# Moving a 16-column GpSimd copy behind eight other instructions, and ScalarE's wait for it to the end of the previous window, in an attention, FFT and FFN kernel

## What is computed

```python
def _moe_ref(x, w_ch1, w_ch2):
    X = np.fft.fft(x, axis=1)
    X = np.fft.fft(X, axis=2)
    mixed = np.real(X).astype(np.float32)
    u = x + mixed
    ...
    un = (u - mu) / np.sqrt(var + 1e-06)
    ch = np.maximum(un @ w_ch1, 0.0) @ w_ch2
    return (u + ch).astype(np.float32)

def _moe2_ref(x, w_val, conv_w, w_out):
    ...
    for k in range(K):
        gate_pre += conv_w[k][None, None, :] * xp[:, k:k + S, :]
    gate = 1.0 / (1.0 + np.exp(-gate_pre))
    val = x @ w_val
    return (gate * val @ w_out).astype(np.float32)
```

## Time and profile before

| | us |
|---|---|
| median of 3 runs | 617.36 |
| lowest and highest | 616.98, 617.66 |
| the profiled execution | 616.98 |
| its span | 615.2 |
| TensorE busy in the span | 604.8 (98%) |
| VectorE, ScalarE, GpSimd busy | 425.7, 345.6, 342.0 |

### The profile page before, as it was taken

One profiled execution on the slowest core, in us unless ns is written; L12 is line 12 of the kernel. 1 busy time (PEld: TensorE's weight loads), 2 busy tenths in 40 slices (PEclk: granted clock), 3 DMA queues, 4 the chain that ended last, 5 costly groups with the idle time before them and its releaser, 6 DMA issues.

```text
span 615.2 us, 10882 instructions
## 1 busy us (share of the span) xinstructions
PE 604.8 (98%) x3682; PEld 502.5 (82%) x3682; DVE 425.7 (69%) x683; ACT 345.6 (56%) x694; POOL 342.0 (56%) x328
## 2 busy tenths in 40 slices
PE   6899999999999999999999999999999999999998
PEld 3667777777767776999888899999999999988887
DVE  3978888888888885788475566655676666579920
ACT  4877777777777785354444344435444444274242
POOL 4543433333337756146325798883999999234140
PEclk9999999999999999999999999999999999999999
DMA  6942323233233110000321212123222221100102
GB/s 146 235 118 64 91 66 90 69 86 90 67 86 92 49 59 7 0 2 2 103 68 52 69 41 67 62 61 99 69 85 85 85 84 53 35 0 1 69 34 103
DMA packets 28177, 42.21 MB, mean 69 GB/s; under 512 B 3440, under 2 KB 16240, under 8 KB 28144
## 3 DMA queue, kind: packets, MB, share of 16 engines
q1 hardware_dynamic: 26176, 37.38, 20.7%
q0 software_dynamic: 1728, 4.02, 2.7%
q10 hardware_dynamic: 240, 0.39, 0.3%
HBM read 38.63 MB, written 3.15 MB: 68 GB/s over the span
## 4 chain that ended last, share of the span: by engine, by line
PE 95%; DVE 2%; ACT 1%; DMA 1%; POOL 1%; issue 0%; SPq 0%; ACTq 0%; POOLq 0%
PE banks L1876 22%; PE banks L1908 14%; PE banks L1663 12%; PE banks L1680 11%; PE banks L1730 10%; PE banks L1867 6%; PE banks L1990 5%; PE banks L2006 5%; PE banks L1703 2%; PE banks L1813 2%; PE banks L1616 2%; PE banks L1738 1%; PE banks L1853 1%; DMA q_raw<-in_q 1%; PE banks L1622 1%; PE banks L1787 1%
## 5 line engine op out<-in xcount | busy, mean ns | idle before, releaser
L1242 DVE TENSOR_REDUCE row_min<-banks 128x1 f32<-128x768 f32 x96 | 91.8, 956 | 32.0 <-PE banks L1663 31.2
L872 ACT ACTIVATE prob<-banks,row_min 128x768 f32<-128x768 f32 x96 | 87.0, 906 | 29.3 <-DVE row_min L1242 29.2
L1730 PE MATMUL banks<-ident,prob 128*128 128x128 f32 x576 | 79.2, 273 | 1.5 <-ACT probT L374 1.4
L1502 DVE TENSOR_TENSOR partial_sums<-banks,partial_sums 128x384 f32<-128x384 f32 x72 | 40.1, 557 | 50.6 <-PE banks L1908 50.5
L1730 PEld LDWEIGHTS banks<-ident,prob 128*128 128x128 f32 x576 | 68.1, 140 | 6.7 <-issue 1.9
L1680 PE MATMUL banks<-probT,v_in 128*64 128x384 f32 x384 | 69.0, 495 | 0.0
L605 POOL TENSOR_TENSOR k_b<-k_raw,k_a 64x768 fp32r<-64x768 f32 x16 | 29.2, 1827 | 69.9 <-ACT k_a L855 69.8
L1876 PE MATMUL banks<-h_hi,w_hi 128*128 128x512 f32 (+1 forms) x256 | 66.1, 339 | 0.0
L1876 PE MATMUL banks<-h_hi,w_lo 128*128 128x512 f32 (+1 forms) x256 | 65.6, 337 | 0.0
L1876 PE MATMUL banks<-h_lo,w_hi 128*128 128x512 f32 (+1 forms) x256 | 65.4, 337 | 0.0
L374 ACT COPY probT<-banks 128x384 f32<-128x384 f32 x104 | 49.0, 479 | 22.5 <-PE banks L1730 22.2
(11 more groups left out here) (216 smaller groups left out, 1511.3 us busy)
## 6 DMA issues: line engine op xcount, KB each, us to landing
w_stage<-in_moe_w_ch SPq DMA_DIRECT2D x40, 256.0 KB, 2.6
q_raw<-in_q SPq DMA_DIRECT2D x32, 192.0 KB, 3.3
k_raw<-in_k SPq DMA_DIRECT2D x30, 192.0 KB, 3.6
v_in<-in_v SPq DMA_DIRECT2D x16, 192.0 KB, 2.8
w_pair<-in_moe_w_ch SPq DMA_DIRECT2D x6, 512.0 KB, 3.8
w_stage<-in_moe_w_ch SPq DMA_DIRECT2D x6, 512.0 KB, 3.8
out<-y_out SPq DMA_DIRECT2D x11, 256.0 KB, 2.0
seq_tables_sb<-in_dft POOLq DMA_DIRECT2D x6, 386.0 KB, 3.7
```

Of the source, the lines that this page charges most:

```text
L872: act.activation(prob[s % 2][:, :, :], s_tile(s), ACT.Exp, bias=row_min[:, s:s + 1], scale=-1.0, accum_out=row_sum[:, s:s + 1]).then_inc(e ...
L1242: dve.tensor_reduce(row_min[:, s:s + 1], s_tile(s), AX.XY, ALU.min).then_inc(min_ready, 1)
L1502: dve.tensor_tensor(out, product_bank[PRODUCT_BANK[o]], other, ALU.add).then_inc(done, 1)
L1730: op = pe.transpose(bank[:, j * P:(j + 1) * P], prob[tile % 2][:, c, j * P:(j + 1) * P], ident[:, :])
```

## The change

On GpSimd, in window 4 (g == SEAM), `finish_x2(0)` is moved from behind the first `split_w2` to behind the second one. In between lie three `split_w1_pair`, the four sums of `sum_w1_pair` and one `split_w2`. On ScalarE, three waits that stood in window 5 ahead of `first_tap(0, 0)` now stand at the end of window 4, which is ahead of `copy_first(5)`. No instruction that computes is added or removed.

```diff
                 split_w2(PLAIN + 2 * g, 0)
-                if g == SEAM:
-                    finish_x2(0)
                 if more:
                     for o in range(4, 7):
                         split_w1_pair(g + 1, o)
                 if g + 2 < WINDOWS:
                     sum_w1_pair(g + 2)
                 split_w2(PLAIN + 2 * g + 1, 1)
+                if g == SEAM:
+                    finish_x2(0)
                 if g > SEAM:
                     split_wvo(g - SEAM - 1)
...
                 copy_first(g)
                 if more:
                     round_w1_pair(g + 1, 0)
-                if g == SEAM + 1:
-                    act.wait_ge(taps_spread, 2)
-                    act.wait_ge(x2_lead, 2)
-                    act.wait_ge(unsum_lo_done, 8)
                 if g > SEAM:
                     first_tap(0, g - SEAM - 1)
...
                 split_w2(PLAIN + 2 * g + 1, 1, PLAIN // 2 + g + 1)
                 if SEAM < g <= SEAM + KB:
                     round_x2(0, slice(g - SEAM - 1, g - SEAM))
+                if g == SEAM:
+                    act.wait_ge(taps_spread, 2)
+                    act.wait_ge(x2_lead, 2)
+                    act.wait_ge(unsum_lo_done, 8)
```

## The result

The changed kernel takes 625.07 us (624.51 to 625.20) against 617.32 us (616.98 to 617.66) before: a ratio of 1.0124, 95% interval 1.0106 to 1.0141, so 7.75 us more. Both are medians of four runs; the 617.36 above is that of three. The prediction was 621.5 us, with a range of 620.7 to 624.4: the direction was right, the time lies above the range. The profiled execution of the changed kernel took 624.13 us, its span is 622.5 us.

The account below looks back on a forecast made before the run. TensorE, busy 98% of the span, was taken as the bound. Copy end 435.09 plus a 1.16 us chain, less 432.07, gave a 4.18 us stall; on the 617.36 median 621.54, forecast 621.5 us, range 620.7 to 624.4.

Parts of the forecast that it names:

- The place, the chain and the sign: Window 4 to 5: late GpSimd copy delays copy_first(5), VectorE's first addition, then TensorE's product 2; slower, chance 0.95.
- The gap: TensorE ahead of product 2 of window 5: stands still 4.18 us, from 432.07 to 436.25; bounds 3.50 and 5.07.
- The handoff from ScalarE to VectorE: Between copy_first(5) and VectorE's first addition of window 5: 0.04 us, estimated from another handoff.
- No second stall: Product 3 of window 5: its addition ends at 438.16, before 438.36; no second wait, or at most 0.2 us.
- The clock: TensorE behind the idle time in window 5: clock taken as unchanged, no loss added to the forecast; chance 0.62.
- rival 1: TensorE behind the idle time in window 5: clock falls to the lower level, 1.9 us more, 623.5 us; chance 0.28.
- Its price: Lower clock behind the idle time: half of 3.78 us lost, 1.9 us; with the late bound 7.0 us, 624.4 us.
- Rival 2: GpSimd runs the eight instructions ahead of the copy in about 5 us; stall about 2 us, 619.4 us; chance 0.06.
- Rival 3: The late copy still meets its wait in time; no slower, 617.0 to 617.4 us; chance 0.04.
- The date that I gave for it: Product 2 of window 5 is on time if GpSimd's copy ends by 432.07 - 1.16 = 430.91 us.

Follow-up runs that it names:

- e1: Changed kernel, but ScalarE's three waits back in window 5 ahead of the first tap, so only GpSimd's copy is moved; 623.77 us.
- e5: Changed kernel with GpSimd's copy one place earlier, ahead of the odd split_w2; 623.19 us.
- e8: Changed kernel with one more GpSimd instruction ahead of the copy, a repetition of the odd split_w2; 626.68 us.
- e10: The changed kernel measured and profiled once more, nothing altered; 625.10 us.
- e11: Changed kernel with VectorE's wait for x2_lead moved to the end of window 5, so only ScalarE's wait meets the late copy; 625.66 us.
- e7: Changed kernel with GpSimd's copy three places earlier, between the second and third weight sum; 621.89 us.
- e2: Changed kernel with GpSimd's copy back at its old place, so only ScalarE's waits are moved; 617.90 us.
- e3: Changed kernel, copy still late, with ScalarE's and VectorE's waits for x2_lead put in window 6, where the data is first read; 617.55 us.
- e6: Changed kernel with GpSimd's copy five places earlier, ahead of the four weight sums; 618.79 us.
- e9: Changed kernel with 5 f32 matmuls of zeros on TensorE ahead of product 2 of window 5, filling 4.5 us; 623.17 us.
- e4b: Changed kernel with 8 f32 matmuls of zeros on TensorE ahead of product 2 of window 5, filling 7.1 us; 625.19 us.

## Why the prediction was right or wrong

**The place, the chain and the sign: right.** The copy starts at 435.39 (forecast 434.9; 0.3 of the difference is there at product 0 already), takes 0.20 us (0.2), L676 ahead of it takes 1.26 (about 1.3), the old order's 1.61 being gone with VectorE's taps; the addition starts at 436.34 (435.65), product 2 is the only thing that waits.

**The gap: mis-sized by 0.4 us,** 4.59 against 4.18. Three terms failed. The third low part of 128x256 took 1.05 us where I kept 0.74 from the kernel before: VectorE's three low parts of h took 3.12 in place of 2.60 us and so ran beside it. That is 0.3 us, less 0.1 that the sums gave back. The handoff from ScalarE to VectorE, for which I took 0.04 from another handoff, was 0.20 us (436.14 to 436.34). The one from GpSimd to ScalarE was 0.07 in place of 0.03. Together 0.2 + 0.16 + 0.04 = 0.4 us.

**No second stall: right.** Product 3 had its inputs; what came late behind the gap was TensorE's own rate.

**The clock: the step that failed.** The forecast put the loss of clock behind the gap at nothing. It was 1.66 us in the first profile of the changed kernel and 2.7 in the second. I had given it a chance of 0.28, as rival 1, and it happened in every profile in which TensorE stood still at this place for 1.8 us or more. The argument for leaving it out of the forecast, that no row told of a gap of 4 us in steady work, was true, but the only row that told of any gap, the half rate after the 3.18 us at the start, spoke for it; I should have followed the row that I had. So did the Trainium skill, page "TensorE: Matmul & The Clock Gate", section "Why this matters for your kernels", with its rule that long enough gaps between bursts put the clock back; the traces of the changed kernel, e1, e5, e8, e10 and e11 agree, with 3.2 to 5.8 us of idle time. The gaps that the page warns of are longer than the 1.8 us of e7, after which the clock fell as well; there the measurement decides.

**Its price: too low as an upper end.** I took 1.9 us from the 3.78 us at the start. It was 1.7 in the first profile, and 2.5 to 2.9 where the lower clock lasted 6.8 us (e1, e10, e11). In e8, with 2.2 of its 6.8 us in the gap, it was 2.2. With 4.6 and 2.7 the sum is 7.3 us; on 617.3 that is 624.6, above the 624.4 at which my range ended.

**What is left.** 625.07 is 0.5 us above 624.6. The kernels whose clock held at this place also lie 0.3 to 0.9 us above before plus delay (e2 0.6, e3 0.3, e6 0.8, e9 0.8, e4b 0.9). Part of this is the tail after ScalarE's last instruction, 2.2 us in the profiled executions of before, e1 and e3 and 2.8 to 3.3 in all others. Whether it is chance which of the two a kernel gets was not tried, and stays open. Another part can be a lower clock elsewhere, as near the start in e7. Where it fell in a timed run is not known, but of the runs of the kernel before on the chip of e1 the five with a mean clock under 1.00 have a median of 618.3 us and the fourteen others 617.0.

**The rivals.** Rival 2, a part that is covered, is out: GpSimd took 7.3 us for the eight instructions (428.09 to 435.39), not 5. Rival 3, a wait met in time, is out too. The date that I gave for it, 430.91, was 0.2 us too late. In e6 the copy, 5 places earlier, ended at 432.38, which is 431.02 if product 0 is put where it was before, and TensorE was still 0.3 us late: that makes the date 430.7. The 0.2 us are those of the two handoffs.

## What to carry to other kernels

A small instruction that others wait for is worth as much as its place in the queue: ask what each wait on it holds back, on every engine, and not only on the one whose wait was moved; here VectorE's unmoved wait made a gap of 3.9 us by itself (e1). Put a wait where the data is first read (e3: the same late copy at no cost). And where a bottleneck engine is made to stand still in steady work, add the lower clock behind the gap to the sum, not to the rivals; here it came with every such gap of 1.8 us of idle time or more.

## What the runs showed of the hardware

- The granted clock of TensorE fell to 0.50 after gaps of 2.0 to 5.9 us in steady matmul work (1.8 to 5.8 us of idle time), and not after 0.3 us. It stayed there for 3.4 or 6.8 us, for the same kernel once the one and once the other (changed kernel and e10). It can fall within the gap (e10) or over a microsecond behind it (e7).
- f32 matmuls with an operand of zeros kept it at 1.00 through 4.5 and 7.1 us (e9, e4b).
- Near the start of the program the clock was low as well in the profiles of e6, e7 and e11, for 3.4 us. Their product 0 comes at 429.2 to 429.3 us, that of all others at 427.6 to 428.5. TensorE had stood still there for 1.78 us up to 12.85 (e7), but it had for as long up to 12.81 in the changed kernel, whose clock did not fall. What decides between the two is open. The stretches of e11:

```profile
13.00:14.00 1.00, 1.00 (x8) 0.68 (x12) 0.12 (x1) 0.00 (x0) 1.00 (x1) 0.97 0.00 0
14.00:16.00 2.00, 2.00 (x11) 0.89 (x4) 1.40 (x2) 0.99 (x2) 0.67 (x1) 0.50 0.42 98
16.00:18.00 2.00, 2.00 (x11) 1.97 (x10) 1.13 (x2) 0.21 (x1) 0.00 (x0) 0.66 0.98 264
```

- The low part of 128x512 on GpSimd took 1.26 us with VectorE idle and 1.61 where part of it ran beside a tap. The copy of 16 columns took 0.20 us with VectorE idle and 0.53 beside the low parts of h. The Trainium skill, page "GPSIMD Engine Reference", section "Specifications", has the rule that the two share their SBUF interfaces; these numbers agree with it.
